# The identity transposes between the steps of the expert routing are left out

## The reference

```python
# 1 attention, 8 heads of 64: only scores within tau of the row's maximum count
scores = scale * q @ k.T
scores = where(scores >= max(scores) - tau, scores, -1e9)
x = softmax(scores) @ v                       # heads side by side: 576 x 512 per batch
# 2 token mixing and a two-layer perceptron
u = x + (x.T @ U @ V).T                       # rank 32
x = u + relu(u @ w_ch1) @ w_ch2               # 512 -> 2048 -> 512
# 3 one of 8 experts for each row
logits = x @ w_gate
local_gate = sigmoid(x @ w_local)
for b, s in rows:                             # in order of s
    fresh_e = argmax(logits[b, s])
    e = fresh_e if s == 0 or local_gate[b, s] < 0.5 else prev_e
    prev_e = e
    p = softmax(logits[b, s])
    out[b, s] = p[e] * (relu(x[b, s] @ w1[e]) @ w2[e])   # 512 -> 1024 -> 512
```

## Time and profile before

| | |
|---|---|
| median of 3 runs | 1113.75 us (1113.57 to 1116.05) |
| the profiled execution | 1114.23 us |
| its span, first to last instruction | 1112.5 us |
| mean granted TensorE clock over the span | 0.992 of full speed |
| PE busy | 1057.5 us (95%) |
| DVE, ACT, POOL busy | 512.1, 468.9, 368.0 us |
| routing, from the first step on the gates to the first expert matmul | about 805 to 831 us of the span |

### The profile page before, as it was taken

The page is one execution under the profiler, slowest core; times in us unless marked ns, Lnnn a source line. Parts: engine busy times, 40 slices in busy tenths (PEclk is TensorE's granted clock), DMA queues, the critical chain, the costliest instruction groups (busy, mean ns, idle before and its releaser), DMA issues.

```text
span 1112.5 us, 20105 instructions
## 1 busy us (share of the span) xinstructions
PE 1057.5 (95%) x7139; PEld 922.8 (83%) x7140; DVE 512.1 (46%) x1000; ACT 468.9 (42%) x894; POOL 368.0 (33%) x340
## 2 busy tenths in 40 slices
PE   6999899999989999998999998999979999999996
PEld 5766789999678999977899996999967788878784
DVE  4675544445444444545444452322373534245631
ACT  5775544434454343546434343222123433244531
POOL 4455222633502362350236224179210111111111
PEclk9999999999999999999999999999999999999999
DMA  7877051615433362534234113241064443154611
GB/s 164 189 184 185 32 139 39 164 62 129 131 90 72 106 160 66 129 110 111 46 110 129 66 39 119 101 146 57 5 230 161 162 139 115 55 191 154 217 34 39
DMA packets 110649, 127.26 MB, mean 114 GB/s; under 512 B 67213, under 2 KB 67213, under 8 KB 110544
## 3 DMA queue, kind: packets, MB, share of 16 engines
q1 hardware_dynamic: 104480, 114.54, 36.2%
q0 software_dynamic: 3520, 10.75, 3.0%
q10 hardware_dynamic: 2544, 0.59, 0.2%
HBM read 87.90 MB, written 10.22 MB: 88 GB/s over the span
## 4 chain that ended last, share of the span: by engine, by line
PE 84%; ACT 4%; DMA 4%; issue 3%; DVE 3%; SPq 1%; POOL 0%; POOLq 0%; DVEq 0%; ACTq 0%
PE mlp_banks L697 18%; PE mlp_banks L689 18%; PE p_down L1382 11%; PE p_up L1382 9%; PE aux L647 7%; PE score_banks L623 6%; PE score_banks L630 6%; DMA xg<-mlp_rows,gather_at 2%; DMA mlp_rows<-z_rows 1%; PE p_turn L1402 1%; PE aux L590 1%; PE p_x L1375 1%; ACT et_first L820 1%; DVE stat L939 1%; PE mlp_banks L679 1%
## 5 line engine op out<-in xcount | busy, mean ns | idle before, releaser
L794 ACT ACTIVATE ex<-score_banks,stat 128x576 f32<-128x576 f32 x132 | 97.7, 740 | 178.0 <-DVE stat L939 178.0
L469 POOL CAST w_hi<-stage 128x1024 fp32r<-128x1024 f32 x64 | 66.5, 1039 | 288.4 <-PE mlp_banks L689 241.5
L697 PE MATMUL mlp_banks<-hid_hi,w_hi 128*128 128x320 f32 (+1 forms) x512 | 158.5, 310 | 0.8 <-DVE hid_lo L987 0.8
L689 PE MATMUL mlp_banks<-u_hi,w_hi 128*128 128x320 f32 (+1 forms) x512 | 157.0, 307 | 2.1 <-ACT u_hi L843 1.6
L948 DVE SCALAR_TENSOR_TENSOR ex<-score_banks,stat,ex 128x576 f32<-128x576 f32 x132 | 107.7, 816 | 106.7 <-ACT stat L798 105.6
L474 POOL TENSOR_TENSOR w_lo<-stage,w_hi 128x1024 fp32r<-128x1024 f32 (+1 forms) x70 | 153.9, 2201 | 4.8
L689 PE MATMUL mlp_banks<-u_hi,w_lo 128*128 128x320 f32 (+1 forms) x512 | 151.3, 296 | 0.0
L697 PE MATMUL mlp_banks<-hid_hi,w_lo 128*128 128x320 f32 (+1 forms) x512 | 151.3, 296 | 0.0
L697 PE MATMUL mlp_banks<-hid_lo,w_hi 128*128 128x320 f32 (+1 forms) x512 | 151.3, 296 | 0.0
L689 PE MATMUL mlp_banks<-u_lo,w_hi 128*128 128x320 f32 (+1 forms) x512 | 151.3, 295 | 0.0
L1382 PE MATMUL p_up<-weights,x_upper 128*128 x336 | 110.6, 400 | 4.0 <-issue 4.0
(11 more groups left out here) (237 smaller groups left out, 1963.9 us busy)
## 6 DMA issues: line engine op xcount, KB each, us to landing
stage<-in_moe_w_ch SPq DMA_DIRECT2D x64, 512.0 KB, 3.7
w_raw<-in_moe_w SPq DMA_DIRECT2D x64, 512.0 KB, 5.2
q_tiles<-q_parts SPq DMA_DIRECT2D x30, 320.0 KB, 3.9
q_tiles<-q_parts SPq DMA_DIRECT2D x60, 160.0 KB, 4.2
k_tiles<-k_parts SPq DMA_DIRECT2D x60, 144.0 KB, 3.4
raw_q<-in_q SPq DMA_DIRECT2D x32, 128.0 KB, 3.2
raw_v<-in_v SPq DMA_DIRECT2D x32, 128.0 KB, 2.9
raw_k<-in_k SPq DMA_DIRECT2D x28, 128.0 KB, 2.7
```

The source lines that it names most:

```text
L469: nc.gpsimd.tensor_copy(w_hi[:, n % RING], stage[:, n % 2]).then_inc(w_upper, 1)
L689: last = nc.tensor.matmul(bank[:, 0:w], ch1(a, g, d, c), of[:, d, cols], start=(d == 0 and n == 0), stop=(d == KC - 1 and n == 2))
L697: last = nc.tensor.matmul(bank[:, 0:w], ch2(a, g, q, c), of[:, q, 0:w], start=(q == 0 and n == 0), stop=(q == QUARTER - 1 and n == 2))
L794: nc.scalar.activation(ex_of(n), score_of(n), ACT.Exp, bias=stat[:, n % 4, 0:1], scale=-1.0).then_inc(exp_done, 1)
```

## The change

The helper `keep_busy` and its seven calls are taken out. No wait, no other instruction and no buffer changes.

```diff
     def tensor(pe):
-        def keep_busy(to, count):
-            for _ in range(count):
-                nc.tensor.transpose(to[:, 0:P], ident[:], ident[:])
-
         pe.wait_ge(keep_made, 1)
...
-        keep_busy(p_x, 12)
         pe.wait_ge(made, CONST_ROWS_AT)
         pe.wait_ge(counted, 1)
...
-        keep_busy(p_x, 4)
         pe.wait_ge(tiles_counted, 1)
...
-        keep_busy(p_x, 8)
         pe.wait_ge(slots_ready, 1)
...
-        keep_busy(p_x, 20)
         for part in range(HOT_PARTS):
             pe.wait_ge(hot_ready, part + 1)
...
         last.then_inc(numbers_ready, 1)
-        keep_busy(p_x, 14)
         pe.wait_ge(prob_ready, 1)
...
         turn_x(0, 0)
-        keep_busy(p_down[:, 1], 8)
         pe.wait_ge(tables, 1)
...
             turn_hidden(t)
-            if t == 0:
-                keep_busy(p_down[:, 1], 14)
```

## The result

The changed kernel takes 1119.04 us, the median of 5 runs (1117.27 to 1121.08), against 1113.75 us before (5 runs, 1113.22 to 1117.39). The ratio is 1.0035, with a 95% interval from 1.0022 to 1.0048: slower by about 3.9 us (the two medians are 5.3 us apart). Forecast were 1117.3 us (+3.4 to +3.5) in a range from 1113.5 to 1120.0. The median lies in that range, and 0.4 us above the forecast's own narrower one, which ended at 1118.6; 3.9 us over the kernel before would be 1117.6, inside both. The profiled execution is one of 1120.29 us with a span of 1118.6, somewhat above the median.

What follows compares the result with a forecast made beforehand. PE, busy 95% of the span and 84% of the chain, was taken as the bound. Delay ahead of tile 0 (+2.2), `up` at half clock (+1.7) and tile 1's gain (-0.46) sum to +3.4 us: 1117.3 us, range 1113.5 to 1120.0.

Steps and rivals of the forecast that it cites:

- The 58 fillers of the routing cost nothing: Routing: five filler groups stand in PE's waits for DVE; cost nothing, at most 0.05 us for the last group.
- The 8 beside the loads: After the first turn_x: register loads hide these fillers; gain 0, at most 0.19 us.
- The 14: Ahead of tile 1: loads wait on a full PE queue; removing these fillers gains 0.46 us, bounds 0 and 1.53.
- The clock falls between 811 and 815.5: Routing without fillers: PE has little work, so its clock drops and is low when the real matmuls come.
- Slot transposes at half clock: Routing, on DVE's path: five slot transposes and tiny matmuls slow down, about +0.3 us, bounds 0 and 0.6.
- L1362: One-hot sums, 20 matmuls: at half clock throughout, 4.5 us instead of 3.54, +1.0 us, bounds -0.5 and +1.0.
- L1368: The 20 matmuls after L1362: 2.45 us now, clock perhaps back for part; +1.5 us, bounds 0 and 2.05.
- Tables and loads: Ahead of tile 0: register loads and `up` move by 0.3 + 1.0 + 1.5 - 0.6 = +2.2 us.
- `up` of tile 0 at half clock: First expert matmuls: a 3.4 us spell at half rate loses 1.7 us, bounds 0 and 2.9.
- The rival that the clock doesn't care: Whole routing: clock stays at 1.00 without fillers, only the 0.46 us is gained, 1113.3 us; chance 0.10.
- The rival of a clock that is back before the expert matmuls: Routing sums slow but wake the clock, `up` at full clock: some +0.9, up to +2.2 us; chance 0.22.
- A fall between tiles 0 and 1: Rival: without the 14 the clock falls again, `up` of tile 1 loses another 1.7 us, 1119.0 us; chance 0.15.

Runs made afterwards that it cites:

- no_8_14: Kernel before without its last two filler groups only (8 after the first turn_x, 14 after turn_hidden of tile 0): ratio 1.0013, 1116.6 us.
- out_loads_late: Changed kernel with three of the six register loads ahead of tile 0 moved behind the last tile: ratio 1.0022 to the kernel before, 1117.9 us.
- tail16: Kernel before with 16 more fillers between the last turn_hidden and the last down: ratio 1.0009, 1116.1 us.
- no_route58: Kernel before without the routing's five filler groups only (12, 4, 8, 20, 14): ratio 1.0035, 1120.2 us.
- only20: Changed kernel with one group back, the 20 fillers ahead of the one-hot sums: ratio 1.0026 to the kernel before, 1118.3 us.

## Why the prediction was right, point by point

- *The 58 fillers of the routing cost nothing.* Right for DVE's path: taken out, no DVE step up to the one-hot parts comes sooner or later. Their work for the clock is what the change lost.
- *The 8 beside the loads: 0.* Right. Without them `up` starts no sooner (no_8_14: 4.65 us from turn_x, against 4.70).
- *The 14: a gain of 0.46 us, not the chain's 1.53.* Right in size: 3.41 became 2.94. The queue's limit, on which it rested, came out in the run with longer groups. For the time the two last groups are not worth this gain: without them alone the kernel is no faster (1.0013).
- *The clock falls between 811 and 815.5.* Right, at 814.3, and at 811.7 to 816.8 in the four other traces whose routing is bare up to there, 6.9 to 7.9 us after its first transpose in all five. The prediction counted 15 small matmuls in that stretch; the trace has 17, which changes nothing.
- *Slot transposes at half clock, +0.3.* Wrong: 0.49 us as before, since the clock was still up. The fall came 0.4 us after they had started, and DVE's path did not feel it. In the trace of out_loads_late they ran at half clock, and the first one-hot sum came 0.14 us later.
- *L1362: +1.0.* Right: 4.53 us against 3.54.
- *L1368: +1.5 (bounds 0 and 2.05).* Mis-sized: 4.53 against 2.45, +2.08, the upper bound. I had thought that 4.5 us of busy L1362 would bring the clock back for part of it. It did not, in this trace or in the other three without any group before L1362. This is the step that had the clock wrong.
- *Tables and loads, +2.2 together.* +2.5 was measured. The two errors above, -0.3 and +0.6, partly cancel, and that is luck.
- *`up` of tile 0 at half clock, +1.7.* +1.65, here. But the size changes from execution to execution: 1.4 to 2.7 us in the traces. The term was taken from spells of 3.4 us, the length of all four that the trace of before has ahead of its last matmul; the one in the changed kernel lasted 23.9 us, of which `up` met the last 3.7, and the one over `up` in tail16 lasted 6.8 us. That the size came out to 0.05 us is luck.
- *Sum +3.4.* The three rows of the table give +3.7 us; the ratio gives 3.9, with 2.5 to 5.3 as its interval. The rival that the clock doesn't care, with its 1113.3 us, falls, and so does the rule of the Trainium skill that would have carried it ("TensorE: Matmul & The Clock Gate", section "🔬 Part 4: PE-mode transpose"): transposes do hold this clock, 0.993 with the routing's 58 and 0.984 without them (no_route58, same chip). The rival of a clock that is back before the expert matmuls did not come, in this trace or in the four others with a bare routing; its +0.9 had left out the 0.6 us of slack that the sum takes off, so it should have been +0.3. A fall between tiles 0 and 1 did not come in the profile of after; it did in those of no_8_14 and out_loads_late, 1.4 us each. That is two of the five traces without the 14, and none of the seven with a group there, so the 0.15 was not too much.

Missed was the end of the kernel: PE's 2.5 us wait ahead of the last `down` is a place for a spell that costs 1.3 to 1.5 us, with or without the change, and the prediction had read it only as idle time. Left open is why the spells with all fillers in place come in one execution and not in another, whether the change makes the one at the end more frequent, and what the filler group of 16 there is worth: alone it gave nothing measurable.

## What to carry to other kernels

Idle time of TensorE beside a busy other engine isn't free: here, after a stretch of 4.9 us with 0.96 us of work, the next real matmuls ran at half rate, and the price is paid where they are on the path. Look for the work at a granted clock of 0.50, not for the gap. Cover the gaps of such a stretch from its first on, since the one group that was put back alone (the 20) ran at half clock itself and landed in the path; other subsets were not tried. Keep the covering work below what the queue takes ahead of register loads, and look whether those loads can go: here moving three was worth about as much (0.29%) as the clock (0.35%).

## What the runs showed of the hardware

- A register load behind a row of transposes starts only when 17 pairs of weight load and transpose, 34 instructions, are left of it: 0.06, 0.07, 0.52, 1.17 and 2.04 us of delay with 12, 16, 22, 28 and 36 pairs. That this is the depth of PE's queue is the reading that fits; the limit was expected from one row and is now shown with five.
- Transposes of the identity hold the clock: 0.993 as the mean over the runs with the routing's 58, 0.984 without them (no_route58).
- A busy PE does not always get its clock back at once: in the changed kernel two stretches of 4.5 us, fully busy with 128-column matmuls, did not end a spell of 23.9 us; in only20, 20 transposes did.
- A register load with its arithmetic takes 0.65 us on PE, the first of a row 0.96 us, one after the other, and can't be seen in the busy times; moving three brought `up` of tile 0 forward by 2.0 and 2.1 us in the traces of two kernels.
